# Layer 1 of attention plus two expert layers: seven tiles of 256 and 512 tokens in place of eight of 384, and a prologue of two chunks

## The reference

```python
for t in range(S):
    state = alpha[:, :, t, :, None] * state + einsum('bhd,bhe->bhde', k[:, :, t], v[:, :, t])
    y[:, :, t] = einsum('bhd,bhde->bhe', q[:, :, t], state)
x = y as tokens x 384
x = (sigmoid(x @ w_gate) * (x @ w_val)) @ w_out                # layer 1, inner width 1536
out = max(x @ w1, x @ w2, x @ w3) @ w_out2                     # layer 2, inner width 768
```

## Time and profile before

| | |
|---|---|
| median of 3 runs | 850.75 us (850.42 to 850.93) |
| profiled execution, its own time | 850.66 us |
| its span, first to last instruction | 848.6 us |
| mean granted TensorE clock | 0.999 |
| TensorE matmul busy | 838.0 us, 99% |
| VectorE busy | 389.0 us, 46% |
| ScalarE busy | 280.2 us, 33% |
| GpSimd busy | 74.5 us, 9% |
| layer 1, first gate matmul to first matmul of layer 2 | 27.66 to 544.46 us |

### The profile page before, as it was taken

How to read it: one execution, slowest core, us unless ns; L and a number is a source line. 1 busy time by engine, 2 the same in 40 slices (tenths; PEclk the granted TensorE clock), 3 DMA queues, 4 the chain that set the end, 5 groups by cost and what they waited for, 6 DMA issues and landing times.

```text
span 848.6 us, 17210 instructions
## 1 busy us (share of the span) xinstructions
PE 838.0 (99%) x6997; PEld 773.5 (91%) x6997; DVE 389.0 (46%) x959; ACT 280.2 (33%) x520; POOL 74.5 (9%) x68
## 2 busy tenths in 40 slices
PE   8999999999999999999999999999999999999997
PEld 7899999999999999999999999988888888888886
DVE  8787565555555455466465322323223232232321
ACT  4655333333333333333333334322212122221212
POOL 1000111111111011021021006300000000000000
PEclk9999999999999999999999999999999999999999
DMA  7440210210210210210200103100101001010101
GB/s 287 163 181 3 100 48 2 101 48 2 101 47 2 100 48 2 101 47 2 100 27 23 49 34 113 38 1 0 38 1 37 0 0 37 0 37 0 37 0 39
DMA packets 14461, 42.36 MB, mean 50 GB/s; under 512 B 1984, under 2 KB 5952, under 8 KB 14400
## 3 DMA queue, kind: packets, MB, share of 16 engines
q1 hardware_dynamic: 14336, 41.41, 13.7%
q10 hardware_dynamic: 64, 0.05, 0.0%
HBM read 35.56 MB, written 4.72 MB: 47 GB/s over the span
## 4 chain that ended last, share of the span: by engine, by line
PE 96%; DVE 2%; DMA 1%; issue 1%; ACT 0%; SPq 0%; DVEq 0%
PE ps_gv L1020 35%; PE ps_out L1045 19%; PE ps_gv L1026 18%; PE ps_out L1140 6%; PE ps_sc L1020 6%; PE ps_sc L1026 3%; PE ps_pair L1140 2%; PE ps_pair L994 1%; PE ps_pair L976 1%; PE ps_pair L926 1%; PE ps_sc L947 1%; PE ps_sc L961 1%; PE ps_pair L947 1%; DVE decay L674 0%; DVE rdec L689 0%
## 5 line engine op out<-in xcount | busy, mean ns | idle before, releaser
L1020 PE MATMUL ps_gv<-x_hi,w_hi 128*128 128x384 f32 (+1 forms) x792 | 279.8, 353 | 1.1 <-ACT x_hi L445 1.1
L1020 PE MATMUL ps_gv<-x_hi,w_lo 128*128 128x384 f32 (+1 forms) x792 | 277.2, 350 | 0.0
L1026 PE MATMUL ps_gv<-x_lo,w_hi 128*128 128x384 f32 (+1 forms) x792 | 235.1, 351 | 0.0
L1020 PEld LDWEIGHTS ps_gv<-x_hi,w_hi 128*128 128x128 f32 x792 | 148.8, 188 | 9.6 <-ACT w_hi L445 1.3
L1020 PEld LDWEIGHTS ps_gv<-x_hi,w_lo 128*128 128x128 f32 x792 | 148.9, 188 | 7.5
L1026 PEld LDWEIGHTS ps_gv<-x_lo,w_hi 128*128 128x128 f32 x792 | 146.0, 188 | 9.6
L791 DVE TENSOR_TENSOR h_sb<-act_sb,ps_gv 128x384 f32<-128x384 f32 x96 | 53.2, 554 | 145.7 <-PE ps_gv L1026 145.4
L445 ACT ACTIVATE h_hi<-h_sb 128x384 fp32r<-128x384 f32 x96 | 50.3, 524 | 145.9 <-DVE h_sb L791 145.8
L491 ACT ACTIVATE act_sb<-ps_gv 128x384 f32<-128x384 f32 x96 | 47.2, 491 | 137.0 <-PE ps_gv L1026 137.0
L890 DVE TENSOR_TENSOR probs<-probs,ps_gv 128x512 f32<-128x512 f32 x36 | 24.8, 689 | 137.9 <-PE ps_gv L1026 137.9
L753 DVE TENSOR_TENSOR h_lo<-h_sb,h_hi 128x384 fp32r<-128x384 f32 x96 | 54.3, 566 | 52.0 <-ACT h_hi L445 52.0
(11 more groups left out here) (128 smaller groups left out, 971.4 us busy)
## 6 DMA issues: line engine op xcount, KB each, us to landing
inbuf<-att_in SPq DMA_DIRECT2D x23, 704.0 KB, 4.5
mid<-w SPq DMA_DIRECT2D x12, 576.0 KB, 7.3
inbuf<-att_in SPq DMA_DIRECT2D x23, 256.0 KB, 3.1
inbuf<-w SPq DMA_DIRECT2D x6, 768.0 KB, 4.3
out<-inbuf SPq DMA_DIRECT2D x5, 768.0 KB, 3.5
x_raw<-x_raw SPq DMA_DIRECT2D x46, 24.0 KB, 1.9
out<-inbuf SPq DMA_DIRECT2D x4, 192.0 KB, 2.9
mid<-att_in SPq DMA_DIRECT2D x1, 704.0 KB, 9.1
```

Source lines behind the costliest of these rows:

```text
L1020: mm(bank, w_at(half, f, c + k * P, total=total), x_hi[:, k, 0:w], start=(k == 0 and half == 0), stop=False)
L1026: return mm(bank, w_at(0, f, c + k * P, total=total), x_lo[:, k, 0:w], start=False, stop=(k == KT - 1))
```

## The change

Layer 1 has seven tiles, of 256, 256, 512, 512, 512, 512 and 512 tokens, that is 2, 2, 4, 4, 4, 4 and 4 chunks. Only chunks 0 and 1 are done in the prologue; `unused(10)` becomes `unused(6)`. Chunk 2 uses the buffer of chunk 0, chunk 3 that of chunk 1, and so on; slots 6 and 7 of the ring are free from the start, and only slot 5 waits (it lends its space to chunk 1's probabilities). The steps at which chunks are scanned, scored and added stand in tables; a negative scan step is one in the tile before. Chunks up to 7 are uncrossed, from chunk 8 on crossed. GpSimd scales all chunks but 0 and 1; `rdec` has one buffer in place of two, and recips wait for the chunk before to be scaled. On ScalarE check(0) moves ahead of khs_copy(1), check(1) into f = 0 of tile 0, and split_w1(1) ahead of y_copy(0). recips of chunk 2 move from before layer 1 into f = 0 of tile 0. All four looped programs are written out.

```diff
+SIZES = (256, 256, 512, 512, 512, 512, 512)
+START = tuple(sum(SIZES[:T]) for T in range(TILES + 1))
+FIRST = tuple(t // CH for t in START)
+PRO = FIRST[1]
+TWO = {"scan": (0, 4), "score": (3, 7), "add": ()}
+TIGHT = {"scan": (-4, 0, 4, 6), "score": (1, 3, 6, 8), "add": ()}
+FOUR = {"scan": (-2, 2, 4, 6), "score": (1, 4, 6, 8), "add": (3, 5, 7, 9)}
+STEPS = (TWO, TIGHT, FOUR, FOUR, FOUR, FOUR)
+CROSSED = FIRST[3]
...
+        def chunk_at(T, f, what):
+            for tile, step in ((T, f), (T + 1, f - NF1)):
+                at = STEPS[tile][what] if tile < len(STEPS) else ()
+                if step in at:
+                    return FIRST[tile + 1] + at.index(step)
+            return None
...
 # SyncE
-            load_chunk(2, 0)
-            for f in range(1, RING - 3):
+            for f in range(1, RING):
+                if f != RING - 3:
+                    load_w1(f)
+            load_alpha(2)
+            move_last(0, (0, 2))
+            load_qkv(2)
+            load_w1(RING - 3)
+            load_chunk(3)
+            for f in range(RING, NF1):
                 load_w1(f)
...
+            for T in range(1, TILES - 1):
+                load_chunk(FIRST[T + 1])
+                move_last(T)
+                for C in range(FIRST[T + 1] + 1, FIRST[T + 2]):
+                    load_chunk(C)
...
 # VectorE, prologue
             new_state(0)
-            scans(2, 0)
-            recips(2, 0, range(PAIRS))
-            scale_qk(2)
             masked(1)
-            masked(2, 0, 0)
-            masked(2, 0, 1)
             new_state(1)
-            new_state(2, 0)
             split_w1(1)
-            scans(3, 0)
+            scans(2)
             for k in range(KT):
                 x_rest(k, k, x_of(0, k))
-            recips(3, 0, range(PAIRS))
...
 # VectorE, a step f of layer 1
+                    scanned, scored, added = (chunk_at(T, f, steps) for steps in ("scan", "score", "add"))
+                    if scanned is not None and scanned > PRO:
+                        scans(scanned)
+                    if scored is not None:
+                        masked(scored, 0)
+                        masked(scored, 1)
+                    h, then h_lo of the step
+                    if scored is not None:
+                        new_state(scored)
+                    if scanned is not None:
+                        recips(scanned, range(PAIRS))
+                    if added is not None and crossed(added):
+                        y_add(added)
+                    if T == 0 and f + 2 < NF1:
+                        split_w1(f + 2)
...
 # TensorE, prologue
             outer(1)
-            unused(10, ident, ident)
-            scores(2, 0)
-            transposes(2, 0)
+            unused(6, ident, ident)
             attend(1)
-            outer(2, 0)
-            attend(2, 0)
             unused(12, ident, ident)
```

More of the change, by code:

```diff
@@ L41 @@
 SUB = TOK2 // P
-CHUNKS = CPT * TILES
+CHUNKS = B * S // CH
+BATCH = S // CH
 SB = 64
@@ L676, in scans, with recips @@
                                                      ALU.mult, ALU.add).then_inc(scan_done, 1)
[L678 to L679 removed]
+            def recips(C, pairs):
+                par = C % 2
                 if 0 in pairs:
[L681 to L684 removed]
+                    dve.wait_ge(scan_done, scans_by(C))
+                    if C > 0:
+                        dve.wait_ge(kh_done, 2 * C)
+                    nc.vector.reciprocal(ends(rdec[0:PR], subs(C)), ends(decay[0:PR, par], subs(C))).then_inc(rend_done, 1)
@@ L779, in layer1 @@
                     g = T * NF1 + f
-                    c = f // 3
-                    att = (C0 + c, i) if att_next and c < CPT else None
-                    scanned = first and c == 0
-                    if att and f % 3 == 0 and not scanned:
-                        scans(*att)
-                    elif att and f % 3 == 2:
-                        masked(*att, 0)
-                        masked(*att, 1)
+                    scanned, scored, added = (chunk_at(T, f, steps) for steps in ("scan", "score", "add"))
+                    if scanned is not None and scanned > PRO:
+                        scans(scanned)
+                    if scored is not None:
+                        masked(scored, 0)
+                        masked(scored, 1)
                     dve.wait_ge(val_done, g + 1)
@@ L983, in attend @@
+            def attend(C):
+                par = C % 2
+                first = C % BATCH == 0
                 pe.wait_ge(mask_done, 2 * C + 2)
-                if not (isinstance(i, int) and Cs < CPT):
+                if C >= PRO:
                     pe.wait_ge(y_evac, C)
-                    pe.wait_ge(state_done, states_by(Cs, i))
+                    pe.wait_ge(state_done, states_by(C))
                 else:
-                    if Cs == 2:
-                        pe.wait_ge(y_evac, 1)
@@ L996, in attend @@
                                start=(p < 2 and s == (1 if first else 0)), stop=False, skip_group_check=True)
-                if subs(Cs, i) == 1:
+                if subs(C) == 1:
                     for p in range(PAIRS):
                         for n in range(2):
-                            ins = value(Cs, i, p, n, 0, start=(first and p < 2))
+                            ins = value(C, p, n, 0, start=(first and p < 2))
                 else:
@@ L1034, in product, with out1 @@
                 return ins
-            def out1(Ts, i, f):
-                T = Ts + 2 * i
-                g = T * NF1 + f
-                if f == 0 and not (isinstance(i, int) and Ts == 0):
+            def out1(T, f):
+                g, w = T * NF1 + f, SIZES[T]
+                if f == 0 and T > 0:
                     pe.wait_ge(mid_done, T * KT)
```

648 lines of the change are left out of this document (296 added, 352 removed).

## The result

The changed kernel takes 853.65 us (median of five, 851.96 to 854.71), the kernel before in the same comparison 850.75 (850.42 to 851.15): ratio 1.0033 with a 95% interval of 1.0022 to 1.0045. It is slower, by about 2.9 us. The profiled execution is the fastest of the five, 851.96 us with a span of 850.2, 1.3 above the profiled one of before.

The account below looks back on a forecast made before the run. TensorE, busy 99% of the span, was taken as the bound. From 850.66 us, -6.0 (prologue) - 3.3 (matmuls) + 4.4 (chunks, joints) + 7.3 (VectorE waits) = +2.4 gave 853.0 us, range 847.8 to 856.

Parts of the forecast that it names:

- parts 1 and 2: Prologue of two chunks starts h(0) earlier, -6.0 us; seven tiles with fewer, wider matmuls after h(0), -3.3 us.
- part 4: VectorE late in tiles 0 and 1: TensorE waits at f=2, 6, 10 and for a tile 1 mask, +7.3 us.
- Rival A: Tile 0: GpSimd does not hold VectorE where it matters, late stretches total 3.7 us; 849.4 us, chance 0.17.
- Rival B: Tile 0: VectorE's splits never make TensorE wait, all of part 4 goes; 845.7 us, chance 0.13.
- D: Matmuls of 256 columns: weight loads show through at 125 ns, 3.2 us more; 855 us, chance 0.07.
- E: All matmuls: the fixed cost per matmul is really small, so part 2's gain goes; 856.4 us, chance 0.03.
- Rival C: GpSimd's second k also holds the w split after the recips, 0.73 us at three places; 855.2 us, chance 0.13.
- One of the prediction's own signs of being wrong: No TensorE wait in tile 0, layer 1 starting after 24 us, or a 512 tile waiting over 0.3 us.
- part 3: Chunk 2 inside layer 1, chunks 6 and 7 uncrossed, and x splits late at tile joints: +4.4 us in all.

Follow-up runs that it names:

- The kernel in which VectorE scales: The changed kernel with VectorE, not GpSimd, scaling q and k of chunks 2 and 3: 850.03 us, ratio 0.9995 to the kernel before.
- the one with the split first: The changed kernel with VectorE splitting w of f+2 before the step's recips in tile 0, not after: 850.08 us, ratio 0.9993 to the kernel before.
- the kernel with the weights behind the moves: A kernel combining several follow-up edits, altered to issue w1 for slots 6 and 7 after the moves and chunk 2's q, k, v: 848.07 us.
- the kernel with chunk 2 early: The changed kernel with chunk 2's alpha, q, k, v issued ahead of the moves and recips(2) ahead of tile 0's x_lo: 850.84 us, ratio 1.0006.

## Why the prediction was right, and where it was not

The direction was right, and so was its cause: waits of TensorE for VectorE in tiles 0 and 1 (7.4 us), which together with the chunk that layer 1 takes over (3.4) outweigh what the shorter prologue and the wider matmuls win (9.2). The gains of parts 1 and 2 came as worked out (first gate 22.52 against 22.4 predicted, 120.0 ns at 256 columns), and so did the four waits of part 4, in place, cause and size: 3.1, 1.6, 1.6 and 1.1 us against 3.3, 1.5, 1.5 and 1.0. In the first of them the sum was right with its parts wrong: q was to hold h_lo(0) for 1.0 us and k the reverse scans for 0.5; measured, h_lo(0) was not held at all and the scans lost 1.26. The kernel in which VectorE scales shows the hold in them, the one with the split first shows VectorE's sum. Rival A is out: the holds are in the trace. Rival B is out: TensorE waits where it said there would be no wait. D and E are out by the 120.0 ns. The formula cited for E, which the page gives for a matmul without its weight load, would give 109.2 ns at 256 columns; the measured ones (120.0, 173.3, 226.7) keep their 13.3 ns over the columns.

Rival C was wrong by its own condition. The split started at 30.24 and GpSimd's second k at 30.40, and it was GpSimd that waited (1.76 us), not the split (1.33). The same at f=6 (48.25 and 48.41) and f=10 (66.26 and 66.42). That a split can be held, when GpSimd is first, the kernel with the weights behind the moves shows (2.45 us). The Trainium skill has the rule that I lacked, on another page than the one I cited ("SBUF — State Buffer", SBUF: two separate sides): whichever of a VectorE operation with two SBUF inputs and a GpSimd operation that reads SBUF starts first has the shared pair for its whole length, and the other is blocked. The traces agree: h_lo, begun 0.14 us after GpSimd's q of 1.30, took 1.44 in place of 0.43.

One of the prediction's own signs of being wrong came up: a 512 tile with a wait of over 0.3 us. It is the start of tile 2, where x is 512 wide and ScalarE does x_hi(0), h_hi and x_hi(1) in the order that part 3 gives. The wait for x_hi is 0.58 us and the whole joint costs 0.92; part 3 had 0.43. The mechanism was there and its size was half.

Two numbers were off and nearly cancelled. First, the term of +4.4 us (chunks and joints) was +3.4. The steps of the two timelines say where, taking each step's length less its 27 matmuls and less the four waits. The 21 chunks inside layer 1 cost TensorE 68.1 us in the kernel before, the 22 of the change 71.0. That is +3.0, where the prediction had 3.45 for chunk 2 and twice 0.25 for chunks 6 and 7. Chunk 2 cost 3.4, but chunks 3 to 5 fell from 3.5 to 3.4 each, chunk 7 rose by 0.1 only, and the sixteen crossed ones took 50.9 us in place of 51.4; why these are cheaper no run shows. The joints cost 0.8 more than before, where the prediction had 0.4. And 0.3 us less lie behind the last matmul, which starts 1.9 us later than before in a span that is 1.6 longer. With 0.3 less around the span the profiled execution is 851.96 and not 853.0. Second, the clock: nothing in the prediction says what TensorE's idle time does to its own clock. In 11 of 17 executions its mean was 0.998 or less, in the one of them that was profiled it fell after the wait ahead of f=2, and the median lies 1.7 us over the fastest. So 853.0 met 853.65 in part by luck, and the reader should take from this case the terms, not their sum. The prediction's own evidence had no case of it: before, TensorE never stood for more than 1.1 us in layer 1.

What stays open: why one execution keeps the clock and the next, with the same wait, does not. The profiled execution that kept it stood 2.93 us at one piece, the one that lost it 0.49 and then 2.55 with one group of nine between. No run here separates these. Nor does the length of the longest wait decide it: the kernel with chunk 2 early has none over 1.0 us from the first gate matmul on and a clock of 0.997 or 0.998 in 5 of 11 executions, the kernels with the split first and with VectorE scaling have one of 1.5 or 1.7 and none in 10 each. Of the change's other parts none was run by itself in the kernel before; their sizes are read from the traces.

## What to carry to other kernels

When tiles are made smaller, list for each engine what does not shrink with the tile (here splits of weights, scans, state updates) and compare the sum with the new length of a step; the excess comes out as waits, and the order decides whose name they bear and in part how much of it TensorE sees. Work handed from VectorE to GpSimd is not free relief: it holds those operations of VectorE with both operands in SBUF that start while GpSimd's runs, and here giving it back shortened tile 0 by 2.15 us in one kernel and by 1.3 in another. Behind a removed wait stands the next (here x_lo, a sigmoid, a mask); look for it in the trace before adding up.
